# A reordered prelude and a second product that follows two steps behind the first, in a window-attention and two-stage MLP kernel

## The reference

```python
scores = scale * np.matmul(q, k.transpose(0, 1, 3, 2))
mask = (rel >= 0) & (rel < window)            # window = 64
attn = softmax(np.where(mask, scores, -1e9))
x = (attn @ v), heads joined: [1152, 512]
...
h = x @ w_in                                  # [512, 2048]
g = np.maximum(h, 0.0) + np.log1p(np.exp(-np.abs(h)))
x = g @ w_out                                 # [2048, 512]
...
p = domain_probs / domain_probs.sum(-1)
for e in range(4):
    h = np.maximum(x @ w1[e], 0.0)            # [512, 1024]
    out += p[:, e:e + 1] * (h @ w2[e])
```

## Time and profile before

| what | value |
|---|---|
| median of three runs | 665.19 us |
| the profiled execution | 665.14 us, of which the span from the first to the last instruction 663.4 us |
| PE busy | 649.6 us (98%) |
| DVE, ACT, POOL busy | 283.1, 227.5, 112.1 us |
| mean granted TensorE clock | 0.992 |
| PE busy from 53.48 us to the end | 606.62 of 609.92 us |
| PE busy from 0 to 53.48 us | 42.95 of 53.48 us |

### The profile page before, as it was taken

The page is one execution under the profiler, slowest core; times in us unless marked ns, Lnnn a source line. Parts: engine busy times, 40 slices in busy tenths (PEclk is TensorE's granted clock), DMA queues, the critical chain, the costliest instruction groups (busy, mean ns, idle before and its releaser), DMA issues.

```text
span 663.4 us, 9932 instructions
## 1 busy us (share of the span) xinstructions
PE 649.6 (98%) x3688; PEld 603.8 (91%) x3688; DVE 283.1 (43%) x677; ACT 227.5 (34%) x573; POOL 112.1 (17%) x103
## 2 busy tenths in 40 slices
PE   7879999999999999999999999999999999999998
PEld 6669999999999999989898989898989898989896
DVE  3676565568646576612151512151512151512121
ACT  4766655557544565402040402040402040402020
POOL 3676633323333334000000000000000000000000
PEclk8889999999999999999999999999999999999999
DMA  8362510033000030300030300030300030110101
GB/s 353 127 251 97 192 64 0 2 126 127 2 1 0 1 119 10 127 1 1 0 126 1 126 1 1 0 126 0 126 0 0 0 126 0 63 47 0 47 0 47
DMA packets 11280, 40.55 MB, mean 61 GB/s; under 512 B 2288, under 2 KB 2288, under 8 KB 9840
## 3 DMA queue, kind: packets, MB, share of 16 engines
q1 hardware_dynamic: 11248, 40.13, 16.7%
HBM read 37.77 MB, written 2.36 MB: 60 GB/s over the span
## 4 chain that ended last, share of the span: by engine, by line
PE 94%; DMA 2%; DVE 2%; ACT 1%; issue 0%; SPq 0%; POOL 0%
PE ps L657 25%; PE ps L688 20%; PE ps_pT L657 10%; PE ps_score L657 10%; PE ps_score L688 10%; PE ps L673 8%; PE ps_score L673 4%; PE ps_o L673 4%; PE ps_score L618 2%; DMA unit_in<-in_units 2%; PE ps_pT L644 1%; PE ps_pT L631 1%; ACT prob L332 1%; DMA raw_a<-in_w_in 1%; DVE rowsum L458 0%; DVE prob L451 0%
## 5 line engine op out<-in xcount | busy, mean ns | idle before, releaser
L657 PE MATMUL ps<-xy_hi,wa_hi 128*128 128x384 f32 (+1 forms) x320 | 110.0, 344 | 0.5 <-DVE xy_lo L466 0.5
L657 PE MATMUL ps<-xy_hi,wa_lo 128*128 128x384 f32 (+1 forms) x320 | 107.8, 337 | 0.0
L657 PE MATMUL ps<-xy_lo,wa_hi 128*128 128x384 f32 (+1 forms) x320 | 107.7, 337 | 0.0
L411 ACT ACTIVATE hid_hi<-ps 128x384 fp32r<-128x384 f32 x48 | 23.6, 492 | 241.7 <-PE ps L657 241.6
L288 POOL TENSOR_TENSOR sp_c<-sp_e,sp_c 128x384 f32<-128x384 f32 x48 | 64.6, 1346 | 118.2 <-DVE sp_c L474 118.2
L688 PE MATMUL ps<-wb_hi,hid_lo 128*128 128x512 f32 x192 | 74.9, 390 | 0.0
L688 PE MATMUL ps<-wb_lo,hid_hi 128*128 128x512 f32 x192 | 74.9, 390 | 0.0
L688 PE MATMUL ps<-wb_hi,hid_hi 128*128 128x512 f32 x192 | 74.7, 389 | 0.0
L657 PEld LDWEIGHTS ps<-xy_hi,wa_hi 128*128 128x128 f32 x320 | 60.6, 189 | 2.5 <-ACT xy_hi L348 0.8
L597 DVE SCALAR_TENSOR_TENSOR part<-ps,gate,part 128x512 f32<-128x512 f32 x24 | 18.0, 751 | 104.8 <-PE ps L688 104.8
L657 PEld LDWEIGHTS ps<-xy_lo,wa_hi 128*128 128x128 f32 x320 | 60.5, 189 | 0.4
(11 more groups left out here) (115 smaller groups left out, 1260.3 us busy)
## 6 DMA issues: line engine op xcount, KB each, us to landing
unit_in<-in_units SPq DMA_DIRECT2D x9, 1024.0 KB, 5.5
raw_a<-in_w SPq DMA_DIRECT2D x16, 512.0 KB, 4.4
raw_b<-in_w SPq DMA_DIRECT2D x16, 512.0 KB, 3.8
raw_a<-in_w_in SPq DMA_DIRECT2D x8, 512.0 KB, 4.7
raw_b<-in_w_out SPq DMA_DIRECT2D x8, 512.0 KB, 4.3
out_dram<-part SPq DMA_DIRECT2D x9, 256.0 KB, 2.0
part<-in_units SPq DMA_DIRECT2D x2, 1024.0 KB, 14.0
unit_in<-in_units SPq DMA_DIRECT2D x1, 640.0 KB, 4.3
```

The costliest lines, as they stand in the source:

```text
L411: act.activation(hid[0][:, f, :], up_banks[f % 4][:, 0:CH], ACT.Relu).then_inc(h_hi, 1)
L657: m = pe.matmul(bank[:, 0:CH], wa[a][:, f, k, :], xy[x][:, bass.ds(c, 1), k, :], start=(k == 0 and i == 0), stop=(k == KT - 1 and i == 2))
```

## The change

Line numbers of before are those of the listing above. The change does the following.

- LAG is 2: `down_width` of step k runs in step k + 2, and the last two of them (before: three) stand between the first products of expert 0.
- The banks follow: units up to 9 alternate between two banks for the transposed probabilities and for the weighted values (`ALT_UNITS` = 10), units up to 11 between two for the scores (`ALT_SCORED` = 12). The first `down_width` waits until `x_low` of unit 9 is done.
- PE's prelude is written out anew: the second transpose and weighing stand one place earlier relative to the scores, transpose 0 stands ahead of the scores of unit 3, transpose 6 ahead of the first start-up product, transpose 7 ahead of the third. In steps 0 and 1 the transpose of unit s + 8 stands ahead of the first product.
- SP brings the queries and keys of the first two groups ahead of their values, and slots are handed on in another order (`slot_of`), so that group 5 waits for unit 1 in place of unit 5, and group 6 for unit 3.
- Weight tiles 4 to 7 are no longer split in the prelude but in iterations 0, 1, 3 and 4 of the loop (`LATE_SPLIT`): one more cast on DVE and one more subtraction on POOL in each. In POOL's loop `normalise` moves ahead of the `wb_lo` subtraction. In the prelude the cast on DVE now stands ahead of `row_inverse`.
- ACT issues `x_high(7)` ahead of the exponentials of unit 9, and copies the transposes of units 8 and 9 ahead of `absolute`.

```diff
-LAG = 3
+LAG = 2
+ALT_UNITS = 8 + LAG
+ALT_SCORED = 10 + LAG
...
         def slot_of(g):
-            return g if g < SLOTS + EARLY else g % SLOTS
+            return g if g < SLOTS + EARLY else (g - SLOTS - EARLY) % SLOTS
...
         def o_bank(u):
-            if u >= UPC:
+            if u >= ALT_UNITS:
                 return ps_pT
-            return ps[2] if u < N_ALT and u % 2 else ps_o
+            return ps[2] if u % 2 else ps_o
...
-        UP_SPLIT = {3: (0,), 4: (1,), 6: (2,), 8: (3,), 9: (4,), 10: (5, 6, 7)}
+        UP_HI = {4: (0,), 5: (1,), 6: (2,), 7: (3,)}
+        UP_LO = {4: (0,), 5: (1,), 6: (2,), 9: (3,)}
+        LATE_SPLIT = {0: 4, 1: 5, 3: 6, 4: 7}
...
             for k in range(STEPS):
                 lost(k // FT, k % FT)
+                if k + SCORED < N_UNITS:
+                    normalise(k + SCORED)
                 if k < FT:
                     pool.wait_ge(wb_hi, k + 1)
                     pool.tensor_tensor(wb[1][:, k, :], raw_b[:, k // 2 % 2, k % 2, :],
                                        f32(wb[0][:, k, :]), ALU.subtract).then_inc(wb_lo, 1)
-                if k < N_UNITS - SCORED:
-                    normalise(k + SCORED)
+                if k in LATE_SPLIT:
+                    up_low(LATE_SPLIT[k])
...
             masked_scores(0)
-            for j in range(UPC + 3):
-                if j + 1 < UPC:
+            masked_scores(1)
+            row_inverse(0)
+            row_inverse(1)
+            masked_scores(2)
+            for j in range(2, SCORED):
+                if j + 1 < SCORED:
                     masked_scores(j + 1)
                 if j >= 3:
                     x_low(j - 3)
-                if j < SCORED:
-                    row_inverse(j)
...
+                if j == SCORED - 1:
+                    x_low(UPC - 1)
+                for f in UP_HI.get(j, ()):
+                    up_high(f)
+                row_inverse(j)
...
-                if u > UPC:
+                if u > ALT_UNITS:
                     pe.wait_ge(x_lo, u)
...
+                if n == 0 and f == 0:
+
+                    pe.wait_ge(x_lo, ALT_UNITS)
+                    pe.wait_ge(negmax_done, ALT_SCORED - 1)
...
+            scores(0)
+            scores(1)
+            scores(2)
+            transpose_probs(0)
+            for j in range(2, UPC - 1):
+                scores(j + 1)
+                transpose_probs(j - 1)
+                weigh_values(j - 2)
+            scores(UPC)
+            transpose_probs(UPC - 2)
+            start_up(0, 0)
+            weigh_values(UPC - 3)
+            scores(UPC + 1)
+            start_up(0, 1)
+            transpose_probs(UPC - 1)
+            start_up(1, 0)
+            weigh_values(UPC - 2)
+            start_up(1, 1)
+            weigh_values(UPC - 1)
             for s in range(STEPS):
                 n, f = s // FT, s % FT
                 c = n % NCH
+                if s < LAG:
+                    transpose_probs(s + WEIGHED)
...
-                if s + WEIGHED < N_UNITS:
+                if LAG <= s < N_UNITS - WEIGHED:
                     transpose_probs(s + WEIGHED)
```

More of the change, by code:

```diff
@@ L35 @@
 EARLY = 2
+SPLIT_GROUPS = 2
 Q_COLS = 2 * 3 * P
@@ L136, in two_stage_mlp_after_window_attention @@
         unit_landed = [sem(f"unit_landed{i}") for i in range(SLOTS + EARLY)]
-        first_landed = sem("first_landed")
+        scores_landed = [sem(f"scores_landed{g}") for g in range(SPLIT_GROUPS)]
         gate_in = sem("gate_in")
@@ L294, in clear_sums, with up_low @@
                 pool.memset(part[:, c, :], 0.0).then_inc(acc_zero, 1)
-            for j in range(UPC + 3):
-                if j < SCORED:
[L298 to L303, removed]
+            def up_low(f):
+                pool.wait_ge(wa_hi, f + 1)
+                pool.tensor_tensor(wa[1][:, f, :, :], raw_a[:, f // 2 % 2, :, P * (f % 2):P * (f % 2) + P],
+                                   f32(wa[0][:, f, :, :]), ALU.subtract).then_inc(wa_lo, 1)
+            for j in range(SCORED):
+                normalise(j)
+                for f in UP_LO.get(j, ()):
+                    up_low(f)
             for k in range(STEPS):
                 lost(k // FT, k % FT)
+                if k + SCORED < N_UNITS:
+                    normalise(k + SCORED)
                 if k < FT:
@@ L378, in y_high @@
                                ACT.Copy).then_inc(y_hi, 1)
-            for j in range(UPC + 3):
-                if 2 <= j < UPC + 2:
+            for j in range(SCORED):
+                if j >= 2:
                     copy_pT(j - 2)
@@ L527, in _, with up_high @@
             dve.wait_ge(consts, N_CONSTS)
+            def up_high(f):
+                dve.wait_ge(raw_a_in[f // 2 % 2], 16 * (f // 4 + 1))
+                dve.tensor_copy(wa[0][:, f, :, :],
+                                raw_a[:, f // 2 % 2, :, P * (f % 2):P * (f % 2) + P]).then_inc(wa_hi, 1)
             masked_scores(0)
-            for j in range(UPC + 3):
-                if j + 1 < UPC:
+            masked_scores(1)
[4 more added lines that the diff above has]
+                if j + 1 < SCORED:
                     masked_scores(j + 1)
@@ L695, in _, with start_up @@
                 pe.matmul(ps[0][:, 0:P], warm[:, :], warm[:, :], start=True, stop=True)
-            STARTS = {UPC - 1: ((0, 0),), UPC: ((0, 1), (1, 0)), UPC + 1: ((1, 1),)}
-            started = [p for products in STARTS.values() for p in products]
-            scores(0)
-            for j in range(UPC + 3):
-                if j + 1 < UPC:
-                    scores(j + 1)
-                if 2 <= j < UPC + 2:
-                    transpose_probs(j - 2)
-                if j >= 3:
-                    weigh_values(j - 3)
-                if UPC <= j + 1 < SCORED:
-                    scores(j + 1)
-                for f, k in STARTS.get(j, ()):
-                    pe.wait_ge(wa_hi, f + 1)
-                    pe.wait_ge(wa_lo, f + 1)
-                    up(up_bank(f), f, 0, True, (k,))
+            STARTED = ((0, 0), (0, 1), (1, 0), (1, 1))
+            def start_up(f, k):
+                pe.wait_ge(wa_hi, f + 1)
+                pe.wait_ge(wa_lo, f + 1)
+                up(up_bank(f), f, 0, True, (k,))
+            scores(0)
+            scores(1)
[16 more added lines that the diff above has]
+            weigh_values(UPC - 1)
             for s in range(STEPS):
@@ L726, in _ @@
                     pe.wait_ge(bank_read, before_in_bank(s))
-                up(up_bank(s), f, c, n < NCH, [k for k in range(KT) if n > 0 or (f, k) not in started])
-                if s + WEIGHED < N_UNITS:
+                up(up_bank(s), f, c, n < NCH, [k for k in range(KT) if n > 0 or (f, k) not in STARTED])
+                if LAG <= s < N_UNITS - WEIGHED:
                     transpose_probs(s + WEIGHED)
```

70 lines of the change are left out of this document (39 added, 31 removed).

## The result

Over 20 runs each the changed kernel takes 666.12 us (665.31 to 668.37), the kernel before 665.18 (663.99 to 665.98). The ratio is 1.0021, with a 95% interval of 1.0015 to 1.0028: slower by 0.2%, where 662.9 was forecast. The profiled execution of the changed kernel took 665.31 us, with a span of 663.5 us and a mean clock of 0.997; before it was 665.14, 663.4 and 0.992. Two single executions lie far off, 1069 us in experiment 5 (mean clock 0.557) and 3649 us in experiment 8, and no ratio counts them.

What follows compares the result with a forecast made beforehand. TensorE, busy 98% of the span, was taken as the bound, with gains only before step 4: 53.48 - 53.57 + 2.29 = 2.20, so 665.14 - 2.20 = 662.94 us, said as 662.9. Range 660.8 to 665.9; likeliest case alone 662.0 to 663.9.

Steps and rivals of the forecast that it cites:

- The formula: At step 4 of the loop: gain is 53.48 - B + 2.29 us, 2.29 being one more second product done by then.
- the fixed amount of work behind step 4: From 53.48 us to the end: a fixed amount of TensorE work as long as no wait is added.
- Up to transpose 5, and to the loop: Prelude: transpose 0 1.4 us earlier, transpose 5 0.95 earlier, weighing 7 at 30.6, DVE entering the loop 3.2 earlier.
- The removed stall: DVE's 2.09 us wait for a weight DMA before the loop goes, and nothing takes its place.
- The first iterations: Loop iterations 0 and 1 lengthen as DVE and POOL block each other; iteration 1 takes 6.5 us, before 5.17.
- TensorE in steps 1 to 3: The 2.99 us idle goes, a 3.5 us wait on x_low(9) comes, 1.7 for slow clock; gain 2.20.
- B: Start of step 4 of the loop after the change, forecast at 53.57 us; it was 53.48 before.
- the gain at step 4: Time won by the start of step 4, counting the extra second product: 2.20 us.
- From step 4 on ... Both cost nothing: Loop from step 4: hid_lo slack stays above 1 us, the first MLP's end keeps its order; both cost nothing.
- DMAs hidden before stay hidden: Prelude: inputs of group 5 and later are not late, and no DMA wait hidden before comes to show.
- The rival with the other sign: Slower: late splits make iterations 1, 3 and 4 take 7.5 us; gain -1.4, 666.5 us; chance 0.11.

Runs made afterwards that it cites:

- experiment 5: The changed kernel run again, not edited, for a second trace: 666.15 us median of 12 runs, ratio 1.0012 against the kernel before.
- experiment 8: The kernel before with LAG = 2 and the first transfer of the second half's second weights moved earlier in SP's queue: 664.48 us, ratio 0.9985.
- experiment 2: The changed kernel with, in SP's queue alone, the second half's first second-weights DMA ahead of the last first-weights DMA: 660.91 us, ratio 0.9937 against before.
- Experiment 10: The changed kernel with the second half's first second-weights DMA earlier in SP's queue and POOL's low split ahead of normalise: 659.56 us, ratio 0.9911 against before.
- experiment 1: The changed kernel with the split of the second half's second weights one iteration later on ACT and DVE: 660.93 us, ratio 0.9935 against the kernel before.
- Experiment 4: The changed kernel with the second half's second-weights split one iteration later and weight tiles 4 to 7 split in iterations 2 to 5: 659.59 us, ratio 0.9921.
- 7: The kernel before with LAG = 2 and nothing else (old prelude, old banks): 668.63 us, ratio 1.0052 against the kernel before.
- 11: The changed kernel with late splits in iterations 2 to 5, the earlier transfer in SP's queue, and POOL's low split ahead of normalise: 660.51 us, ratio 0.9927.

## Why the prediction was wrong, step by step

- **The formula and the fixed amount of work behind step 4** hold but for 0.2 us. In experiment 2 the formula gives 4.28; with the 2.08 us that the second product takes at the end of the first MLP it gives 4.07, and 4.13 is measured there.
- **Up to transpose 5, and to the loop**: 10.15, 21.65 and 30.6 forecast for transpose 0, transpose 5 and weighing 7; 10.41, 21.87 and 29.55 measured. The removed stall went as said: mask 10 at 32.50, forecast 33.1.
- **The first iterations**: 5.15 and 6.20 us, forecast 5.6 and 6.5; masks 11 and 12 at 37.65 and 43.85, for 38.7 and 45.2. Blocking between DVE and POOL is there, on the operations that the prediction named. Experiment 10 shows it by moving one of them. Two readings behind this part were wrong, without effect on the sum. The row for an operation with a PSUM input, x_low at 44.44, shows nothing, since POOL was idle from 44.29; the row 43.34 of the same trace does, 0.54 us beside POOL's 42.97 to 44.29. And "no POOL operation is longer than 1.32" is not so: L288 has a mean of 1.346 us.

```profile
43.34 0.54 DVE L480 SCALAR_TENSOR_TENSOR sp_l<-ps,sp_l 128x384 f32<-128x384 f32 x1
```

- **TensorE in steps 1 to 3**: the forecast wait on x_low ahead of the first second product, 3.5 us, came as 3.25. Four traces have that wait, of 3.15 to 3.25 us. Half rate follows it in two (experiments 1 and 5) and not in the other two (the changed kernel and experiment 2). Without it x_low of unit 10 decided step 4, as the prediction says: TensorE waited 0.94 us at transpose 11. B was 52.27 in place of 53.57 since x_low of unit 10 ended at 48.43 in place of 49.6. Nearly all of that is the earlier mask 10 (0.6) and the shorter iterations (0.75). In experiments 2 and 5 step 4 came another 0.8 and 1.05 earlier; their clock from 10 to 15 us was 1.00, where the changed kernel's first trace has 0.66. In experiment 1 half rate lasted longer (clock 0.56 and 0.75 in the windows 40 to 45 and 45 to 50), and step 4 came at 52.92. So the gain at step 4 was mis-sized: 3.5 to 4.6 in three of these traces and 2.85 in the fourth, for 2.20. With the transfer mended the time is 660.9, at the low end of the range. This error is 2 us and points away from the one that decided.
- **"From step 4 on ... Both cost nothing" is the step that failed.** It looked at the slack of `hid_lo` against the second product in a steady iteration, and at the end of the first MLP. It did not look for the other places where LAG sets an iteration: the split of the second half's weights moved from iteration 20 to 19, and its transfer did not. An earlier sentence, "DMAs hidden before stay hidden", was argued for the attention inputs alone and fails here. The row that warned of it was to be had: ACT's 2.83 us wait on that very DMA in the kernel before, hidden by slack. With LAG 2 ACT needs the same transfer one step earlier, 4.2 us at this place, and the second product behind it has one step less of slack. The term put at nothing costs 3.45 us in the one trace of the changed kernel and 5.3 in the other (experiment 5). Experiments 1 and 2 take it away from either end, and 7 and 8 bring it into the kernel before and take it away again.
- **The rival with the other sign** had its loss in the late splits. Experiment 4 shows that they do cost, 1.3 us, but that is not what made the kernel slower.

What stays open is why an idle stretch of some 3 us is followed by half rate in one execution and by full rate in another of the same kernel. Its length alone does not say it: ahead of the first second product the changed kernel idled for 3.25 us in its first trace, with full rate behind it, and for 3.15 in experiment 5, with half rate. Open too is how the 5.2 us between the medians of the changed kernel and of 1 or 2 divide. That they are the wait and mostly the half rate behind it is argued from one profiled execution of two and from the one run at clock 1.000. A rival stays: the transfer took 4.2, 4.6 and 6.9 us from its issue to ACT's cast in the three traces in which PE waited for it, so a longer transfer in the executions that were not profiled could make up a part. Both are costs of the same late transfer.

## What to carry to other kernels

When a constant that sets the distance of two steps is changed, look up every place that uses it, and for each follow the inputs of the moved work back to the queue that brings them: a wait that was hidden before (here 2.83 us of ScalarE on a DMA) is the first candidate. A gain measured at one point of a timeline holds only if the rest has no wait, so walk the rest as well. And where VectorE and GpSimd both work, try GpSimd's long operations beside those of VectorE that read PSUM, but look at what then comes last in GpSimd's queue: it gave 1.35 us in experiment 10 and cost 1.1 in 11, where that last operation was needed sooner.

## What the runs showed of the hardware

- One late transfer can cost more than its wait: 3.65 us of idle TensorE were followed by matmuls at half the pace until 151.2, 1.7 us more. In another execution of the same kernel 3.20 us of idle were followed by clock 1.00. In the thirteen traces of this case TensorE idles for 2.96 us or more 12 times (after the first 12 us); half rate follows 9 times, full rate 3 times. The Trainium skill (TensorE: Matmul & The Clock Gate, section "Part 1: The HAM clock gate (the "warmup" mystery)") says of a kernel's start that the same kernel shows another number of slow matmuls from run to run; the rows here show such a difference deep within a kernel.
- A VectorE operation of 128x384 with two SBUF inputs takes 0.55 us by itself and 1.16 us when a GpSimd operation of 0.83 us has begun 0.08 us before it; the three such operations shown above end 0.41 to 0.42 us after the GpSimd operation beside them. The same shape with one PSUM input is not held up: in experiment 2 it took 0.55 us at 39.95, wholly within GpSimd's 1.31 us from 39.58.
